# Reordering the start: tile 1's first state in step 1, products within tiles 0 and 1 by even and odd heads, a gate subtraction behind the finishes

## Chip, cores and metric
One core of one Trainium2 chip runs the whole program in one launch. The metric is the device time of a launch in microseconds; lower is better. Engines: TensorE multiplies matrices (PE in profile rows, PEld its weight loads), VectorE (DVE) and ScalarE (ACT) work elementwise, GpSimd (POOL) does elementwise work and masks, SyncE (SP) issues the DMAs.

## The reference
Three layers in a row, all in float32. The first is a gated linear recurrence over 768 positions for 2 batches of 8 heads of width 40:

```
m_new = max(f_t + m, i_t)
C = exp(f_t + m - m_new) * C + exp(i_t - m_new) * v_t k_t^T
n = exp(f_t + m - m_new) * n + exp(i_t - m_new) * k_t
y_t = sigmoid(o_t) * (C q_t) / max(|n . q_t|, 1)
```

The second scales y (1536 tokens of 320 numbers) by its inverse root mean square and a gain, and computes `(silu(x @ w_gate) * (x @ w_val)) @ w_out` with an inner width of 1536. The third is `leaky(x @ w_in) @ w_out` with an inner width of 2048 and a slope of 0.01 for negatives.

## The kernel before
The tokens are cut into 12 tiles of 128, n = 0 to 11, two of them (one for each batch) for each stretch of 128 positions. Tiles 0 and 1 are the first of their batch and have no earlier state. The recurrence is done by chunks. For a tile, the score products `k q^T` of each head (`scores`, L1092) are multiplied by a table of decays (VectorE, L802), and `within` (L1131) multiplies that by the values. Each tile also leaves a state (`update_state`, L1121), which later tiles of its batch use (`from_state`). VectorE divides by the denominator (`denominator`, L841 to L844, and `finish`, L850 and L855), ScalarE squares and normalises (L574, L580, with an inverse root on GpSimd, L456, between them), and TensorE turns the tile (`turn`, L1144 and L1147) into the layout in which the second layer reads it. VectorE and ScalarE split the turned values into a high and a low part (`x_hi`, `x_lo`, `x_odd`; L863 to L888, L589, L596), since products are done in a format of fewer bits.

The second layer is a list of steps (`STEPS`), each a block of 128 of the 1536 inner columns for 2 or 4 tiles. Step s has `gate(s)` and `value(s)`, eight products each of 256 or 512 columns (L1166), then tanh on ScalarE (`first1`, L619), `gated` (L908), `hidden1` (L915), `high1` (L633) and `low1` (L929) on VectorE and ScalarE, and `out1` on TensorE (L1205, L1209) one or two steps later. Steps 0 to 9 are for tiles 0 and 1. The recurrence of tiles 2 to 11 runs beside the steps, at places that the table `BESIDE` gives: tile 2's scores go before gate(2).

The weights come by DMA into a ring of three tiles (`raw`), ScalarE rounds them into the high part (L613, `hi_weights`), and GpSimd subtracts to get the low part (L483, L485, `lo_weights`). gate(s) waits for its low part.

Each engine has one hand-written order, and semaphores join them. In the start, TensorE has: exponents of tiles 0 and 1, scores(0), scores(1), within(0), within(1), two tables of gate sums for the later tiles (`table`, L1056: five transposes each of 16 rows), update_state(0), the last rows of the sums (L1270), turn(0), turn(1), update_state(1), gate(0), value(0), gate(1), value(1). The tables land in PSUM and are taken by `later_tables` on VectorE: L780 copies the sums into `a_tab`, L783 subtracts them and gives `c_tab`, which ScalarE's decays of tile 2 on need (L551). L968 makes the input of the second table; it stands on VectorE between the last score product of tile 1 and the first denominator.

`p_done` counts the score products of VectorE, two for each tile: z = 0 for the even heads, z = 1 for the odd. `dc_done` counts the state updates, `tab_ps` the tables in PSUM, `tab_done` the tables in SBUF, `exp_tab` the exponentials of them, `a_done` the gate sums, `gate_used` the runs of `gated`. The states of tiles 0 and 1 lie in two parts of the PSUM bank `c_ps`; `first_state` copies them to SBUF (L821), and scores(2), which write `c_ps` too, wait for both copies. SyncE loads the q and k of tile n into the place of tile n - 2 and waits for `dc_done` n - 1 before it.

Of the kernel before, what the change touches and what calls it, by code (L numbers as in the profile page):

```python
# [8 lines left out]
ALU = mybir.AluOpType  # L9
# [6 lines left out]
SEQ_TILES = S // P  # L16
# [75 lines left out]
def build(nc, first_gates, gates, qk, tok, w1, w2, consts, scratch, out):  # L92
    ctx = ExitStack()
    with ctx:
# [213 lines left out]
        def width(s):  # L308
            return STEPS[s][1] * P if s < STEPS1 else CHUNK
# [229 lines left out]
        def _(act):  # L539
# [131 lines left out]
            nc.scalar.activation(ea_tab[:, NG:], a_tab[:, NG:], ACT.Exp).then_inc(exp_tab, 1)  # L671
            act.wait_ge(tab_ps, 4)
            for z in range(2):
# [65 lines left out]
        def _(dve):  # L739
# [37 lines left out]

            def later_tables():
                dve.wait_ge(tab_ps, 2)
                nc.vector.tensor_copy(a_tab[:, NG:], later_a_ps).then_inc(tab_done, 1)  # L780
                dve.wait_ge(tab_ps, 3)
                dve.wait_ge(tab_done, 2)
                nc.vector.tensor_tensor(c_tab[:, NG:], later_c_ps, a_tab[:, NG:], ALU.subtract).then_inc(tab_done, 1)  # L783
# [31 lines left out]
            def first_state(n):  # L815


                dve.wait_ge(dc_done, FIRST)
# [146 lines left out]
            for n in range(FIRST):  # L965
                for z in range(2):
                    scores(n, z)
            nc.vector.tensor_tensor(ig[0:NG, rest], ig[0:NG, rest], m, ALU.subtract).then_inc(a_done, 1)  # L968
            for n in range(FIRST):
                denominator(n)  # L970
                finish(n)
            later_tables()
            first_x_high()
# [3 lines left out]
            first_state(0)  # L977
            first_state(1)

# [3 lines left out]
            for s in range(1, STEPS1 + 1):  # L983
# [5 lines left out]
                if s < STEPS1:  # L989
                    gated(s, width(s))  # L990
                if h_first(s):
                    hidden1(s, width(s))
# [58 lines left out]
        def _(pe):  # L1051
# [74 lines left out]
            def within(n):  # L1126
                pe.wait_ge(tok_in[n % 2], 16 * (n // 2 + 1))
                pe.wait_ge(p_done, 2 * n + 2)
                for h in range(H):
# [135 lines left out]
            table(later_a_ps, acum, 1, SEQ_TILES)  # L1265
            pe.wait_ge(a_done, 4)
            table(later_c_ps, ig, 1, SEQ_TILES)
            update_state(0)
            pe.wait_ge(tab_done, 3)
# [3 lines left out]
            update_state(1)  # L1273

            gate(0)
            value(0)
            for s in range(1, STEPS1 + 1):
# [3 lines left out]
                if s < STEPS1:  # L1281
                    gate(s)
                for n in work["R"]:
                    from_state(n)
                    within(n)
                    update_state(n)
# [6 lines left out]
                if s == RING:  # L1293

                    pe.wait_ge(exp_tab, 2)
                for ready in outs(s):
                    out1(ready)
# [71 lines left out]
```

## Time and profile before

| | |
|---|---|
| time, median of 3 runs | 440.34 us (439.75 to 440.49) |
| the profiled execution | 440.19 us, span 438.5 us |
| TensorE busy | 429.8 us, 98% of the span |
| VectorE, ScalarE, GpSimd busy | 226.3, 193.3, 91.0 us |

The span runs from the first to the last recorded work of the profiled execution; the rest of its own time lies around the span. All rows below are of that one execution, and times in them count from the start of the span. A timeline row gives the start, the duration of the merged group, the engine, the line, the operation, what it writes and reads, and, in brackets, how long the engine idled before it and what ended the wait. Ends of TensorE's rows are modelled, and neighbouring products overlap, so spacings are taken from starts.

### The profile page before, as it was taken

To read this page: it belongs to the slowest core of one execution; us is meant where nothing else is said; L and a number is where in the kernel's file an instruction comes from. 1 tells how busy PE (TensorE), PEld (TensorE's weight loads), DVE (VectorE), ACT (ScalarE), POOL (GpSimd) and SP (SyncE) were. 2 spreads that over 40 slices of the span, in tenths; PEclk is the share of its full clock that TensorE was granted. 3 is DMA by queue.
4 is the path that set the end of the run, shared out by engine and by line. 5 is a ranking of instruction groups with operands and counts; after the bars stand their busy time and mean duration, and the time that the engine had idled before them with its cause. 6 is when DMAs were issued, how large, how long until landed. Compare 5 with 4: busy or idle time off the path is not lost.

```text
span 438.5 us, 8229 instructions
## 1 busy us (share of the span) xinstructions
PE 429.8 (98%) x3237; PEld 377.7 (86%) x3237; DVE 226.3 (52%) x439; ACT 193.3 (44%) x428; POOL 91.0 (21%) x97
## 2 busy tenths in 40 slices
PE   7999999999999999999999999999999999999997
PEld 5889999999788888878888888989999999999996
DVE  8856656775466555456433335353333333533534
ACT  4867753665262535235333226553343343333332
POOL 1798852212111111002333004430000000000000
PEclk9999999999999999999999999999999999999999
DMA  7887623431202410001222102300000000100101
GB/s 213 279 294 257 215 86 124 126 121 51 78 27 98 131 47 0 1 1 33 66 67 66 34 1 67 100 0 1 0 1 0 1 1 1 44 17 0 61 0 60
DMA packets 10692, 30.42 MB, mean 69 GB/s; under 512 B 1296, under 2 KB 3264, under 8 KB 10656
## 3 DMA queue, kind: packets, MB, share of 16 engines
q1 hardware_dynamic: 10656, 29.92, 21.4%
q8 instruction: 25, 0.41, 0.4%
q14 instruction: 11, 0.09, 0.1%
HBM read 27.90 MB, written 2.01 MB: 68 GB/s over the span
## 4 chain that ended last, share of the span: by engine, by line
PE 82%; issue 6%; POOL 4%; DMA 4%; DVE 3%; ACT 1%; SPq 0%; POOLq 0%; DVEq 0%
PE gate_ps L1166 22%; PE value_ps L1166 22%; PE out_ps L1243 9%; PE out_ps L1205 9%; PE turn_ps L1243 6%; PE out_ps L1209 3%; PE c_ps L1243 3%; PE turn_ps L1131 3%; POOL w_sb L483 2%; DMA raw<-in_w 2%; PE turn_ps L1092 1%; DMA att_sb<-in_tok 1%; PE turn_ps L1109 1%; PE c_ps L1121 1%; DMA y_acc<-in_first_gates 1%
## 5 line engine op out<-in xcount | busy, mean ns | idle before, releaser
L1166 PE MATMUL value_ps<-x_hi,w_sb 128*128 128x512 f32 (+1 forms) x280 | 68.6, 367 | 0.5 <-DVE h_lo L929 0.5
L1166 PE MATMUL gate_ps<-x_hi,w_sb 128*128 128x512 f32 (+1 forms) x280 | 68.8, 368 | 0.2
L1166 PEld LDWEIGHTS gate_ps<-x_hi,w_sb 128*128 128x128 f32 x280 | 47.4, 191 | 8.2 <-DVE x_odd L895 1.1
L1166 PEld LDWEIGHTS value_ps<-x_hi,w_sb 128*128 128x128 f32 x280 | 47.7, 191 | 7.4 <-DVE h_lo L929 0.7
L908 DVE SCALAR_TENSOR_TENSOR act_buf<-act_buf,gate_ps 128x512 f32<-128x512 f32 (+1 forms) x46 | 26.2, 569 | 48.1 <-ACT act_buf L619 47.9
L934 DVE TENSOR_TENSOR h_lo<-hid,h_hi 128x512 fp32r<-128x512 f32 x48 | 33.2, 692 | 33.7 <-ACT h_hi L638 33.7
L633 ACT ACTIVATE h_hi<-value_ps 128x512 fp32r<-128x512 f32 (+1 forms) x46 | 23.0, 500 | 58.4 <-DVE value_ps L915 58.2
L1205 PE MATMUL out_ps<-h_hi,w_sb 128*128 128x512 f32 (+1 forms) x184 | 48.2, 348 | 0.0
L638 ACT ACTIVATE h_hi<-hid 128x512 fp32r<-128x512 f32 x48 | 30.3, 632 | 37.6 <-DVE hid L922 36.5
L619 ACT ACTIVATE act_buf<-gate_ps 128x512 f32<-128x512 f32 (+1 forms) x46 | 23.1, 501 | 49.3 <-PE gate_ps L1166 49.1
L1243 PE MATMUL out_ps<-w_sb,h_hi 128*128 128x320 f32 x192 | 43.0, 309 | 0.2 <-DVE h_lo L934 0.2
L491 POOL TENSOR_TENSOR w_sb<-raw,w_sb 128x704 fp32r<-128x704 f32 x16 | 27.4, 1716 | 76.0 <-ACT w_sb L613 76.0
L1166 PE MATMUL gate_ps<-x_lo,w_sb 128*128 128x512 f32 (+1 forms) x140 | 39.3, 362 | 0.0
L1166 PE MATMUL value_ps<-x_lo,w_sb 128*128 128x512 f32 (+1 forms) x140 | 39.2, 362 | 0.0
L1166 PE MATMUL gate_ps<-x_odd,w_sb 128*128 128x512 f32 (+1 forms) x140 | 39.1, 361 | 0.0
L1166 PE MATMUL value_ps<-x_odd,w_sb 128*128 128x512 f32 (+1 forms) x140 | 39.0, 360 | 0.0
L915 DVE SCALAR_TENSOR_TENSOR value_ps<-act_buf,value_ps 128x512 f32<-128x512 f32 (+1 forms) x46 | 26.5, 577 | 22.2 <-PE value_ps L1166 22.0
L929 DVE TENSOR_TENSOR h_lo<-value_ps,h_hi 128x512 fp32r<-128x512 f32 (+1 forms) x46 | 26.5, 575 | 19.7 <-ACT h_hi L633 19.5
L1205 PEld LDWEIGHTS out_ps<-h_hi,w_sb 128*128 128x128 f32 x184 | 31.7, 190 | 3.8
L922 DVE SCALAR_TENSOR_TENSOR hid<-gate_ps,act_buf 128x512 f32<-128x512 f32 x24 | 16.6, 691 | 34.7 <-ACT act_buf L626 34.7
L1243 PEld LDWEIGHTS out_ps<-w_sb,h_hi 128*128 128x128 f32 x192 | 32.7, 188 | 1.8 <-DVE h_lo L934 0.6
L922 DVE SCALAR_TENSOR_TENSOR hid<-value_ps,act_buf 128x512 f32<-128x512 f32 x24 | 16.6, 691 | 30.4 <-ACT act_buf L626 30.4
(148 smaller groups left out, 797.5 us busy)
## 6 DMA issues: line engine op xcount, KB each, us to landing
raw<-in_w SPq DMA_DIRECT2D x12, 544.0 KB, 4.6
att_sb<-in_tok SPq DMA_DIRECT2D x12, 484.0 KB, 4.8
raw<-in_w SPq DMA_DIRECT2D x16, 352.0 KB, 3.0
expo<-decay_scratch SPq DMA_DIRECT2D x10, 512.0 KB, 5.3
att_sb<-in_qk SPq DMA_DIRECT2D x24, 160.0 KB
out_y<-y_acc SPq DMA_DIRECT2D x12, 160.0 KB, 1.9
consts_sb<-in_consts SPq DMA_DIRECT2D x1, 129.5 KB, 2.7
y_acc<-in_first_gates SPq DMA_DIRECT2D x1, 112.0 KB, 2.6
```

The lines of the kernel that those rows point to most:

```text
L491: nc.gpsimd.tensor_tensor(w[:, W2RAW:W2], r, w[:, 0:W2RAW].bitcast(F32), ALU.subtract).then_inc(w_lo, 1)
L619: nc.scalar.activation(act_buf[:, s % RING, 0:n], gate_ps[:, 0:n], ACT.Tanh, scale=0.5)\
L633: nc.scalar.activation(h_hi[:, r, cols], value_ps[:, 0:width(s)], ACT.Copy).then_inc(hi_done, 1)
L638: nc.scalar.activation(h_hi[:, r, :], hid[:, r, :], ACT.Copy).then_inc(hi_done, 1)
L908: nc.vector.scalar_tensor_tensor(out=a, in0=a, scalar=1.0, in1=gate_ps[:, 0:n], op0=ALU.add, op1=ALU.mult).then_inc(gate_used, 1)
L915: nc.vector.scalar_tensor_tensor(out=value_ps[:, 0:n], in0=act_buf[:, s % 2, 0:n], scalar=0.5, in1=value_ps[:, 0:n], op0=ALU.mult, op1=ALU ...
L922: nc.vector.scalar_tensor_tensor(out=hid[:, r, :], in0=in_ps[r][:, :], scalar=0.01, in1=act_buf[:, r, :], op0=ALU.mult, op1=ALU.max)\
L929: nc.vector.tensor_tensor(h_lo[:, r, cols], value_ps[:, 0:width(s)], h_hi[:, r, cols].bitcast(F32), ALU.subtract).then_inc(h_done, 1)
L934: nc.vector.tensor_tensor(h_lo[:, r, :], hid[:, r, :], h_hi[:, r, :].bitcast(F32), ALU.subtract).then_inc(h_done, 1)
L1166: last = nc.tensor.matmul(ps[:, 0:n], lhs, rhs, start=(j == 0), stop=(j == len(xs) - 1))
L1205: nc.tensor.matmul(out_ps[k][:, cols], lhs, rhs[:, r, place], start=(f == 0 and t == 0 and j == 0), stop=(f == NF1 - 1 and j == 2))
L1243: ins = nc.tensor.matmul(y_ps(i, k)[:, 0:DM], lhs[:, r, tok], rhs, start=(f == 0 and j == 0), stop=(f == GF - 1 and j == 2))
```

## The change
On TensorE, `within` of tiles 0 and 1 goes through the even heads first and waits only for the first score product of its tile, then through the odd heads behind the second. `update_state(1)` moves from before gate(0) to between gate(1) and value(1). The second table, of `later_c`, moves from behind the first one to between gate(0) and value(0), and waits there for `exp_tab`, since it shares a bank with the last rows. These waited for three tables in SBUF and now wait for two.

On VectorE, L968 moves behind the finishes of both tiles and the copy of `a_tab`. `later_tables` is cut in two: `later_sums` stays, `later_gates` goes behind the copy of tile 0's state. That copy waits for tile 0's update alone, and tile 1's copy moves behind gated(1) in step 1. TensorE's wait for `c_tab` moves to before the first `out1`, which writes into that bank.

```
--- before.py
+++ after.py
@@ -669,7 +669,7 @@
             x_high(1)
             act.wait_ge(tab_done, 2)
             nc.scalar.activation(ea_tab[:, NG:], a_tab[:, NG:], ACT.Exp).then_inc(exp_tab, 1)
-            act.wait_ge(tab_ps, 4)
+            act.wait_ge(tab_ps, 3)
             for z in range(2):
                 rows = slice(z * HP, (z + 1) * HP)
                 logs = later_last_ps[rows, :].rearrange("p (m z) -> p z m", z=2)[:, z, :]
@@ -775,10 +775,12 @@
             nc.vector.tensor_tensor_scan(acum[0:NG, rest], restart[0:NG, rest], f, 0.0, ALU.mult, ALU.add)\
                 .then_inc(a_done, 1)
 
-            def later_tables():
+            def later_sums():
                 dve.wait_ge(tab_ps, 2)
                 nc.vector.tensor_copy(a_tab[:, NG:], later_a_ps).then_inc(tab_done, 1)
-                dve.wait_ge(tab_ps, 3)
+
+            def later_gates():
+                dve.wait_ge(tab_ps, 4)
                 dve.wait_ge(tab_done, 2)
                 nc.vector.tensor_tensor(c_tab[:, NG:], later_c_ps, a_tab[:, NG:], ALU.subtract).then_inc(tab_done, 1)
 
@@ -814,8 +816,7 @@
 
             def first_state(n):
 
-
-                dve.wait_ge(dc_done, FIRST)
+                dve.wait_ge(dc_done, n + 1)
                 for p in range(2):
                     rows = slice(p * HP, p * HP + D)
                     ins = nc.vector.tensor_copy(state[rows, n, :], state_ps(n)[rows, 0:PAIRS * DV])
@@ -965,17 +966,17 @@
             for n in range(FIRST):
                 for z in range(2):
                     scores(n, z)
-            nc.vector.tensor_tensor(ig[0:NG, rest], ig[0:NG, rest], m, ALU.subtract).then_inc(a_done, 1)
             for n in range(FIRST):
                 denominator(n)
                 finish(n)
-            later_tables()
+            later_sums()
+            nc.vector.tensor_tensor(ig[0:NG, rest], ig[0:NG, rest], m, ALU.subtract).then_inc(a_done, 1)
             first_x_high()
             for n in range(FIRST):
                 x_low_main(n)
             first_low_odd()
             first_state(0)
-            first_state(1)
+            later_gates()
 
             gated(0, width(0))
             hidden1(0, width(0))
@@ -988,6 +989,8 @@
                     denominator(n)
                 if s < STEPS1:
                     gated(s, width(s))
+                if s == 1:
+                    first_state(1)
                 if h_first(s):
                     hidden1(s, width(s))
                 for n in work["O"]:
@@ -1125,8 +1128,13 @@
 
             def within(n):
                 pe.wait_ge(tok_in[n % 2], 16 * (n // 2 + 1))
-                pe.wait_ge(p_done, 2 * n + 2)
-                for h in range(H):
+                if n >= FIRST:
+                    pe.wait_ge(p_done, 2 * n + 2)
+
+                heads = [*range(0, H, 2), *range(1, H, 2)] if n < FIRST else range(H)
+                for i, h in enumerate(heads):
+                    if n < FIRST and i % PAIRS == 0:
+                        pe.wait_ge(p_done, 2 * n + i // PAIRS + 1)
                     for t0 in range(0, P, HP):
                         last = nc.tensor.matmul(within_ps(n)[t0:t0 + HP, h * DV:(h + 1) * DV],
                                                 expo[:, n % EXPO, h * P + t0:h * P + t0 + HP],
@@ -1263,16 +1271,17 @@
             within(1)
             pe.wait_ge(a_done, 3)
             table(later_a_ps, acum, 1, SEQ_TILES)
-            pe.wait_ge(a_done, 4)
-            table(later_c_ps, ig, 1, SEQ_TILES)
             update_state(0)
-            pe.wait_ge(tab_done, 3)
+            pe.wait_ge(tab_done, 2)
             nc.tensor.matmul(later_last_ps, last_row_sb, a_tab[:, NG:], start=True, stop=True).then_inc(tab_ps, 1)
             turn(0)
             turn(1)
-            update_state(1)
 
             gate(0)
+            pe.wait_ge(a_done, 4)
+
+            pe.wait_ge(exp_tab, 2)
+            table(later_c_ps, ig, 1, SEQ_TILES)
             value(0)
             for s in range(1, STEPS1 + 1):
                 work = beside(s - 1)
@@ -1280,6 +1289,9 @@
                     scores(n)
                 if s < STEPS1:
                     gate(s)
+                if s == 1:
+
+                    update_state(1)
                 for n in work["R"]:
                     from_state(n)
                     within(n)
@@ -1293,6 +1305,7 @@
                 if s == RING:
 
                     pe.wait_ge(exp_tab, 2)
+                    pe.wait_ge(tab_done, 3)
                 for ready in outs(s):
                     out1(ready)
             for g in range(GROUPS):
```

## Rows read from the trace of the kernel before

**Rows 1.** Busy time by stretch: span, each engine, PEclk, DMA share, GB/s
```profile
20.50:24.00 3.50, 3.50 (x20) 3.46 (x17) 2.84 (x9) 2.81 (x9) 3.50 (x4) 1.00 0.98 314
...
27.00:438.40 411.40, 407.42 (x3022) 358.73 (x3020) 205.77 (x387) 175.50 (x381) 75.32 (x72) 1.00 0.18 57
```

**Rows 2.** Timeline of GpSimd: start us, us, operation, [idle before it]
```profile
16.64 0.54 POOL L456 TENSOR_TENSOR ms<-ms,minus_half 128x1 f32<-128x1 f32 x1
...
20.63 0.33 POOL L485 TENSOR_TENSOR w_sb<-raw,w_sb 128x64 fp32r<-128x64 f32 x1
```

**Rows 3.** Timeline of TensorE, 9 to 34 us
```profile
11.93 3.64 PE L1131 MATMUL turn_ps<-att_sb,expo 128*64 128x41 f32 x64 [0.58 <-DVE expo L802]
15.50 1.24 PE L1056 MATMUL out_ps<-consts_sb,y_acc 16*128 16x16 f32 x10
...
19.48 0.42 PE L1147 MATMUL value_ps<-consts_sb,xn 128*64 128x128 f32 x1
19.84 0.78 PE L1121 MATMUL c_ps<-att_sb,kw 128*40 128x41 f32 x16
20.54 1.23 PE L1166 MATMUL gate_ps<-x_hi,w_sb 128*128 128x256 f32 x4
...
22.42 1.06 PE L1166 MATMUL value_ps<-x_hi,w_sb 128*128 128x256 f32 x4
...
24.02 0.64 PE L1166 MATMUL gate_ps<-x_hi,w_sb 128*128 128x256 f32 x4
...
25.65 0.74 PE L1166 MATMUL value_ps<-x_hi,w_sb 128*128 128x256 f32 x4 [0.52 <-DVE h_lo L929]
...
26.80 0.37 PE L1092 MATMUL turn_ps<-att_sb 40*128 40x128 f32 x1
...
33.48 0.49 PE L1121 MATMUL c_ps<-att_sb,kw 128*40 128x41 f32 x16
```

**Rows 4.** Timeline of ScalarE
```profile
15.63 0.47 ACT L574 ACTIVATE xn<-yt 128x321 f32<-128x321 f32 x1 [0.38 <-DVE yt L855]
...
17.63 0.55 ACT L580 ACTIVATE xn<-yt,ms 128x320 f32<-128x320 f32 x1
...
20.48 0.39 ACT L676 ACTIVATE dec_tab<-out_ps 64x40 f32<-64x40 f32 x2
...
22.94 1.27 ACT L551 ACTIVATE expo<-expo,c_tab 128x128 f32<-128x128 f32 x4
```

**Rows 5.** Timeline of VectorE
```profile
11.09 0.69 DVE L802 TENSOR_TENSOR expo<-expo,gate_ps 128x512 f32<-128x512 f32 x1
...
13.33 0.84 DVE L968 TENSOR_TENSOR y_acc<-y_acc 16x640 f32<-16x640 f32 x1
...
16.63 0.49 DVE L855 TENSOR_TENSOR yt<-turn_ps,den 128x320 f32<-128x320 f32 x1
...
17.38 0.24 DVE L783 TENSOR_TENSOR c_tab<-out_ps,a_tab 128x80 f32<-128x80 f32 x1
19.24 0.61 DVE L863 TENSOR_SCALAR x_hi<-out_ps,consts_sb 128x128 fp32r<-128x128 f32 x2 [1.62 <-PE value_ps L1147]
...
21.17 0.48 DVE L888 SCALAR_TENSOR_TENSOR x_odd<-value_ps,consts_sb,x_odd 64x256 fp32r<-64x256 f32 x1
21.68 1.36 DVE L821 COPY state<-c_ps 40x164 f32<-40x164 f32 x4
...
25.59 0.42 DVE L908 SCALAR_TENSOR_TENSOR act_buf<-act_buf,gate_ps 128x256 f32<-128x256 f32 x1
```

**Rows 6.** DMA issued from 10.4 to 11.2 us: count, size, median us to landing
```profile
raw<-in_w SPq DMA_DIRECT2D x1, 544.0 KB, 4.9
```

**Rows 7.** Timeline of SyncE's DMA issues
```profile
10.61 0.43 SPq L374 DMA_DIRECT2D raw<-in_w  x1
...
25.13 0.68 SPq L352 DMA_DIRECT2D att_sb<-in_qk  x2
...
27.32 4.74 SPq L374 DMA_DIRECT2D raw<-in_w  x2
```

More of the change, by code:

```diff
@@ L671, in _ @@
             nc.scalar.activation(ea_tab[:, NG:], a_tab[:, NG:], ACT.Exp).then_inc(exp_tab, 1)
-            act.wait_ge(tab_ps, 4)
+            act.wait_ge(tab_ps, 3)
             for z in range(2):
@@ L776, in _, with later_sums, later_gates @@
                 .then_inc(a_done, 1)
-            def later_tables():
+            def later_sums():
                 dve.wait_ge(tab_ps, 2)
                 nc.vector.tensor_copy(a_tab[:, NG:], later_a_ps).then_inc(tab_done, 1)
-                dve.wait_ge(tab_ps, 3)
+            def later_gates():
+                dve.wait_ge(tab_ps, 4)
                 dve.wait_ge(tab_done, 2)
@@ L815, in first_state @@
             def first_state(n):
-                dve.wait_ge(dc_done, FIRST)
+                dve.wait_ge(dc_done, n + 1)
                 for p in range(2):
@@ L967, in _ @@
                     scores(n, z)
-            nc.vector.tensor_tensor(ig[0:NG, rest], ig[0:NG, rest], m, ALU.subtract).then_inc(a_done, 1)
             for n in range(FIRST):
@@ L971, in _ @@
                 finish(n)
-            later_tables()
+            later_sums()
+            nc.vector.tensor_tensor(ig[0:NG, rest], ig[0:NG, rest], m, ALU.subtract).then_inc(a_done, 1)
             first_x_high()
@@ L977, in _ @@
             first_state(0)
-            first_state(1)
+            later_gates()
             gated(0, width(0))
@@ L990, in _ @@
                     gated(s, width(s))
+                if s == 1:
+                    first_state(1)
                 if h_first(s):
@@ L1127, in within @@
                 pe.wait_ge(tok_in[n % 2], 16 * (n // 2 + 1))
-                pe.wait_ge(p_done, 2 * n + 2)
-                for h in range(H):
+                if n >= FIRST:
+                    pe.wait_ge(p_done, 2 * n + 2)
+                heads = [*range(0, H, 2), *range(1, H, 2)] if n < FIRST else range(H)
+                for i, h in enumerate(heads):
+                    if n < FIRST and i % PAIRS == 0:
+                        pe.wait_ge(p_done, 2 * n + i // PAIRS + 1)
                     for t0 in range(0, P, HP):
@@ L1265, in _ @@
             table(later_a_ps, acum, 1, SEQ_TILES)
-            pe.wait_ge(a_done, 4)
-            table(later_c_ps, ig, 1, SEQ_TILES)
             update_state(0)
-            pe.wait_ge(tab_done, 3)
+            pe.wait_ge(tab_done, 2)
             nc.tensor.matmul(later_last_ps, last_row_sb, a_tab[:, NG:], start=True, stop=True).then_inc(tab_ps, 1)
@@ L1272, in _ @@
             turn(1)
-            update_state(1)
             gate(0)
+            pe.wait_ge(a_done, 4)
+            pe.wait_ge(exp_tab, 2)
+            table(later_c_ps, ig, 1, SEQ_TILES)
             value(0)
@@ L1282, in _ @@
                     gate(s)
+                if s == 1:
+                    update_state(1)
                 for n in work["R"]:
@@ L1295, in _ @@
                     pe.wait_ge(exp_tab, 2)
+                    pe.wait_ge(tab_done, 3)
                 for ready in outs(s):
```

## Prediction

> **What bounds the kernel now.** I read the table of stretches first. From 27 us to the end TensorE is busy for 407.42 of 411.40 us, so whatever happens at the start moves the end by as much as it moves TensorE's first steps, and by nothing more [rows 1]. Behind 27 us it runs through its steps almost without a stop. The weights are no limit either: the weights of `gate(1)` are split by GpSimd at 20.96 and TensorE asks for them at 24.02, 3 us later [rows 2, 3]. So the question is only when the first `gate`/`value` pair and the chain behind it come.
>
> The timeline of TensorE shows the start as a relay. It stands idle for 0.58 and starts `within` at 11.93, when VectorE has both score products of tile 0, and is done with both tiles at 15.57. After the turns (the last one starts at 19.48) it does `update_state(1)` from 19.84, gate(0) from 20.54, value(0) from 22.42, gate(1) from 24.02, and then stands idle for 0.52 before value(1) at 25.65, waiting for VectorE's low part of step 0 [rows 3]. ScalarE's timeline shows why the turns come when they do: behind `hi_weights(1)` it idles 0.38, to 15.63, for tile 0's y, and from there square, weights, square, normalise, normalise run one behind the other up to the last turn [rows 4].
>
> **The clock.** The column of the granted clock reads 1.00 before 24 us and behind 27 alike [rows 1], but four products of 256 columns take 1.06 in value(0) and 0.64 in gate(1) [rows 3]: 0.42 less over three spacings, so 0.213 against about 0.12 each. The first is 256 columns at the 1.2 GHz level, the second nearly that at 2.4 GHz. The rise comes at about 24.0, after 3.5 us in which TensorE did full 128 by 128 products without a pause; `within`, tables and turns before ran at the lower level.
>
> **The change, part by part.**
>
> 1. `within` by even and odd heads. The 64 records take 3.64 us either way. The even heads need only the first product, which is over before the second begins at 11.09 [rows 5], so TensorE can use the 0.58 that it idled: start at 11.35, done at 14.99. The odd heads need the second product (11.78) and come to their turn at 12.26, a quarter of 3.64 later. Bounds: 0 to 0.84 (11.93 less 11.09); I take 0.58, the idle time of the row.
>
> 2. VectorE subtracts behind the finishes. L968 (13.33 to 14.17) leaves the place between the last product and the denominators, so up to 0.84 of VectorE goes ahead of the finishes; but tile 1's needs `within(1)`, so I take the 0.58 of part 1: its y ends at 16.54 instead of 17.12. L968 now lies between about 16.8 and 17.7, inside the 1.62 that VectorE idled until 19.24 for the turned tile [rows 5]; without that cover it would cost 0.84.
>
> 3. What of it reaches the turns. ScalarE is busy with `hi_weights(1)` until 15.25 (15.63 less 0.38), so tile 0's square gains only that idle 0.38 [rows 4]. Behind it come `hi_weights(2)`, whose raw tile was issued at 10.61 and lands 4.9 later, at 15.5 [rows 6, 7], in time for its turn at 15.7 (15.25 and 0.47 for the square), and then square(1) at about 16.8, for which y is ready at 16.54. GpSimd's inverse root for tile 0 ends at 17.18, being held by its own weights [rows 2]; normalise(0), at 17.63 before [rows 4], wants it at 17.25. So 0.38 of the 0.58 passes, and the last turn starts at 19.10.
>
> 4. `update_state(1)` leaves the place before gate(0): 0.70 of TensorE (19.84 to 20.54). But gate(0) then meets its operands. VectorE's chain of low parts ends with L888 at 21.17 + 0.48 = 21.65 [rows 5], which becomes 21.27; gate(0)'s last two products need it, so they start at 21.33, and with 0.05 for the restart gate(0) has issued all at about 21.8. Of 1.08 (0.38 + 0.70) some 0.6 is left. Bounds: 0.38 (only the shift) to 1.08 (no wait for operands), the row of L888 decides.
>
> 5. `table(later_c)` goes between gate(0) and value(0). Ten transposes of both tables take 1.24 at the low clock [rows 3], so five take 0.62, and I add 0.1 for the two changes of kind. In the old place they were hidden, since TensorE waited for normalise afterwards; here they are in front of value(0). The sum: 21.8 + 0.7 = 22.5, against 22.42. Bounds 0.31 (higher clock) to 0.9. Its own waits, for the subtraction (17.7) and for the last-row exponentials (20.87 before, [rows 4], 20.5 now), are satisfied.
>
> 6. `later_gates` (0.24, [rows 5]) follows tile 0's state copies on VectorE: L821 took 1.36 for both tiles, 0.68 for one, so 21.3 to 22.0, then it waits for the table, 22.6 to 22.85. Queued behind it is gated(0), at about 22.9 instead of 23.04 (21.68 + 1.36); the ScalarE decay of tile 2 that needs the c table started at 22.94 [rows 4] and would start about then. Cost 0; a table 0.3 later would begin to delay gated(0), which gate(1) waits for only at 24.0.
>
> 7. `update_state(1)` goes between gate(1) and value(1), in TensorE's idle 0.52. At the higher clock a state update is 0.49 [rows 3], at the lower 0.78. Cost 0 to 0.3; I take 0, as value(1) waits for VectorE's low part until 25.65 anyway. VectorE copies the state behind gated(1) (25.59 + 0.42 = 26.01), to 26.7, while TensorE is in value(1); scores(2), which need that copy, start at 26.80 [rows 3, 5]. Margin 0.1, cost 0 to 0.1.
>
> 8. SyncE: tile 3's q and k wait for the second state update. They went out at 25.13 [rows 7], now at about 25.8, and the issue after them (27.32, weights) waits for GpSimd and not for them. Cost 0.
>
> The sum at value(0) is +0.1 us, and with nothing later changed also at the end. The profiled execution took 440.19 (span 438.5, 1.7 outside it), 0.15 under the median of 440.34. So 440.3 for the execution, 440.4 for the median.
>
> **A rule weighed against the rows.** The rows show five transposes newly placed in the stretch of full products after which the clock rises [rows 3]. The Trainium skill (TensorE: Matmul & The Clock Gate, Part 4) says that PE transposes do not bring TensorE to its full clock as products do. By it this change thins the very work that releases the clock; by the rows alone the rise stays at 24.0. The result of this rule is the first rival, and no row of this trace can confirm it.
>
> **Rivals.**
>
> *The clock rises later (slower).* Place: gate(0) now has pauses for operands, and 0.7 us of small transposes follow it, where before there were 3.5 us of unbroken full products. For it: the mixed work from 11.9 to 20.5 never raised the clock. Against: TensorE is still hardly idle. Price: gate(1) from 24.1 with eight products at 0.213 (1.7), the state update (0.7) and value(1) (1.7) end at 28.2 instead of 26.8: +1.4, so 441.8; the idle 0.52 before value(1) is counted in it. It decides (over 0.88) from a rise later than about 26.5, when over eight products that nothing hides cost 0.093 more each.
>
> *The clock rises earlier (faster).* `within` now follows the scores without the 0.58 pause, so scores, products and tables make one unbroken run. If this, or the earlier gate(0), brings the higher clock by 21.3, then the two last products take 0.24, the table 0.31 and 0.1, value(0) 0.96: it is issued at 22.95 instead of 24.02, less 1.07: 439.3. Against: 3.6 us of `within` without a pause did not do it before.
>
> *The clock follows gate(0) by the same distance as before.* Gate(0) starts 0.85 earlier (19.7, ScalarE's and VectorE's high parts of tile 1 being the 0.38 earlier), so the rise is at 23.1: of value(0)'s products some six, and not the last one or two, save 0.093 each, 0.5; with +0.1 and the median, 440.0.
>
> *The change doesn't do what it says at the front.* TensorE may not start the even heads early, or ScalarE's weights be late: the 0.38 is lost, the table stays: +0.5, 440.8.
>
> **How the numbers follow.** Within 0.2% is 0.88 us, about what a measurement of this kernel can tell. Forecast 0.36 (439.9 to 440.9 by the bounds of parts 4, 5 and 7), clock follows 0.12, front not gained 0.06: together 0.54 within. Clock later 0.24, slower. Clock earlier, or more of the 1.08 of part 4 passing with it, 0.22, faster. The range 439.1 to 441.8 reaches to both outer cases and leaves out their far tails, some 0.15.
>
> **What the profile after would show.** Right: `within` at 11.3 or before, the last turn near 19.1, gate(0) from about 19.7 with a pause before its low products, the table near 21.9, value(0) at 22.5, value(1) near 25.7, and full products at 0.12 from 24.0. Wrong in part 3: the last turn at 18.8 or 19.4. Wrong in part 5: value(0) at 22.1 or before. The number itself fails above all if the spacing of 0.213 ends somewhere else than at 24.0.

## The result, and the profile after

The changed kernel takes 442.45 us (median of 7 runs, 441.34 to 442.80), the kernel before 440.34 in the same measurement: a ratio of 1.0046, with an interval of 1.0036 to 1.0056. It is 2.1 us slower. The forecast was 440.4, the range ended at 441.8. The profiled execution took 442.8, span 441.1.

The table of stretches of the changed kernel, with the columns of [rows 1]:

```profile
20.50:24.00 3.50, 3.50 (x16) 2.96 (x17) 2.59 (x9) 2.35 (x7) 3.50 (x4) 1.00 0.93 280
24.00:29.00 5.00, 5.00 (x37) 4.69 (x37) 1.85 (x6) 3.15 (x11) 3.45 (x4) 1.00 0.79 288
29.00:441.00 412.00, 407.99 (x3026) 358.98 (x3025) 205.87 (x387) 175.52 (x381) 75.19 (x71) 1.00 0.18 56
```

Behind 29 us TensorE is idle for 4.01 us, as it was for 3.98 behind 27 us before [rows 1]. Nothing was lost or won there: the whole difference lies ahead of scores(2). The timeline of TensorE, with the rows that answer to [rows 3]:

```profile
12.03 3.64 PE L1139 MATMUL turn_ps<-att_sb,expo 128*64 128x41 f32 x64
15.60 0.71 PE L1059 MATMUL out_ps<-consts_sb,y_acc 16*128 16x16 f32 x5
...
19.70 0.42 PE L1155 MATMUL value_ps<-consts_sb,xn 128*64 128x128 f32 x1
20.30 1.19 PE L1174 MATMUL gate_ps<-x_hi,w_sb 128*128 128x256 f32 x4 [0.18 <-ACT x_hi L589]
21.46 0.79 PE L1174 MATMUL gate_ps<-x_lo,w_sb 128*128 128x256 f32 x2
22.05 0.71 PE L1174 MATMUL gate_ps<-x_odd,w_sb 128*128 128x256 f32 x2
22.70 0.71 PE L1059 MATMUL out_ps<-consts_sb,y_acc 16*128 16x16 f32 x5
23.34 1.22 PE L1174 MATMUL value_ps<-x_hi,w_sb 128*128 128x256 f32 x4
...
25.21 1.05 PE L1174 MATMUL gate_ps<-x_hi,w_sb 128*128 128x256 f32 x4
...
27.05 0.78 PE L1124 MATMUL c_ps<-att_sb,kw 128*40 128x41 f32 x16
27.76 1.22 PE L1174 MATMUL value_ps<-x_hi,w_sb 128*128 128x256 f32 x4
28.78 0.44 PE L1174 MATMUL value_ps<-x_lo,w_sb 128*128 128x256 f32 x2
...
29.38 0.37 PE L1095 MATMUL turn_ps<-att_sb 40*128 40x128 f32 x1
```

From start to start, after against [rows 3]: gate(0) begins 0.24 earlier; gate(0) to value(0) takes 3.04 instead of 1.88 (+1.16); value(0) to gate(1) 1.87 instead of 1.60 (+0.27); gate(1) to value(1) 2.55 instead of 1.63 (+0.92); value(1) to scores(2) 1.62 instead of 1.15 (+0.47). The sum is +2.58, and the span grew by 2.6.

Four products of 256 columns take 1.05 to 1.22 everywhere from gate(0) to value(1). Before, gate(1) was the first to take 0.64 [rows 3]. The spacing of 0.213, 256 columns at the 1.2 GHz level, now ends in the low products of value(1), at about 28.9 instead of 24.0. The granted clock column reads 1.00 all the while, as it did before, but the trace holds no record of the clock for that time: its first record, at full, begins at 28.86 here and at 23.88 before. The spacings and the first record put the rise at the same place.

The rows that answer to [rows 5] are those of VectorE:

```profile
17.30 0.85 DVE L973 TENSOR_TENSOR y_acc<-y_acc 16x640 f32<-16x640 f32 x1
...
21.44 0.48 DVE L889 SCALAR_TENSOR_TENSOR x_odd<-value_ps,consts_sb,x_odd 64x256 fp32r<-64x256 f32 x1
21.95 0.67 DVE L822 COPY state<-c_ps 40x164 f32<-40x164 f32 x2
23.45 0.24 DVE L785 TENSOR_TENSOR c_tab<-out_ps,a_tab 128x80 f32<-128x80 f32 x1 [0.83 <-PE out_ps L1059]
```

VectorE works in the order that the prediction said, the subtraction some 0.5 later than it said. But `x_odd` ends at 21.92, later than before (21.65), and not at 21.27. In this execution the start itself was late: ScalarE's first half of `raw` waited 0.84 for its DMA and began at 13.44, and GpSimd's inverse root came at 17.30 instead of 16.64:

```profile
17.30 1.27 POOL L456 TENSOR_TENSOR ms<-ms,minus_half 128x1 f32<-128x1 f32 x2
```

That is why I ran the same kernel twice more (below).

### The profile page after: what moved, and what is told of

Its sections match the earlier page's. It is cut to its first block, busy times and chain, and to the rows that moved or that the text cites. A ratio compares the mean times of both kernels' runs of the same rounds, so it can differ in the third digit from the quotient of the medians.

```text
span 441.1 us, 8230 instructions
## 1 busy us (share of the span) xinstructions
PE 432.2 (98%) x3237; PEld 379.0 (86%) x3237; DVE 226.5 (51%) x439; ACT 193.4 (44%) x428; POOL 91.2 (21%) x97
## 4 chain that ended last, share of the span: by engine, by line
PE 82%; issue 6%; POOL 5%; DMA 2%; ACT 2%; DVE 2%; SPq 1%; POOLq 0%; DVEq 0%; ACTq 0%
PE gate_ps L1174 23%; PE value_ps L1174 23%; PE out_ps L1251 9%; PE out_ps L1213 9%; PE turn_ps L1251 6%; PE out_ps L1217 3%; POOL w_sb L483 3%; PE c_ps L1251 3%; DMA raw<-in_w 2%; PE turn_ps L1139 2%; PE turn_ps L1095 1%; PE turn_ps L1112 1%; PE c_ps L1124 1%; POOL w_sb L485 1%; ACT w_sb L613 1%
## 5 line engine op out<-in xcount | busy, mean ns | idle before, releaser
L916 DVE SCALAR_TENSOR_TENSOR value_ps<-act_buf,value_ps 128x512 f32<-128x512 f32 (+1 forms) x46 | 26.6, 577 | 22.9 <-PE value_ps L1174 22.7
L930 DVE TENSOR_TENSOR h_lo<-value_ps,h_hi 128x512 fp32r<-128x512 f32 (+1 forms) x46 | 26.5, 575 | 19.2 <-ACT h_hi L633 18.9
```

Of the source, the lines that this page charges most:

```text
L916: nc.vector.scalar_tensor_tensor(out=value_ps[:, 0:n], in0=act_buf[:, s % 2, 0:n], scalar=0.5, in1=value_ps[:, 0:n], op0=ALU.mult, op1=ALU ...
L930: nc.vector.tensor_tensor(h_lo[:, r, cols], value_ps[:, 0:width(s)], h_hi[:, r, cols].bitcast(F32), ALU.subtract).then_inc(h_done, 1)
```

## The experiments

Three theories: the clock rises later because the small table products stand between gate(0) and value(0) (A in the expectations); or it is the work itself, table, restarts, late operands and state update, at any clock; or the subtraction moved on VectorE disturbs someone else (C in the expectations). The time of the kernel before beside each run was measured together with it. Execution times of one kernel mostly spread by 1 to 3 us, so ratios with their intervals decide, and rows of one execution show only what was possible in it.

**1. The same products, two kinds.** Into the kernel before, between gate(0) and value(0), five unneeded transposes (a repeat of the second table), or three unneeded full products of about the same length. The outputs don't change.

```
             gate(0)
+            pe.wait_ge(exp_tab, 2)
+            table(later_c_ps, ig, 1, SEQ_TILES)
             value(0)
```

> The kernel before, with five more transposes of the second table between gate(0) and value(0) (a second copy of work already done). Theory A, the clock: small transposes break the stretch of full products, the spacing of 0.213 us lasts beyond 24.9 us, and the time grows by 1.3 to 2.5 us. Theory B, only work: the 0.65 us of transposes are added in front of value(0) and nothing else, so +0.6 to +0.8 us, with the spacing of 0.12 from about 24 us.

Measured: 441.22 beside 440.19, ratio 1.0023 (1.0009 to 1.0037), runs from 439.67 to 442.36. That lies between what the two theories expected, and the interval doesn't tell them apart.

```
             gate(0)
+            for _ in range(3):
+                nc.tensor.matmul(out_ps[0][:, 0:FIRST * P], w1_sb[:, 0, 0:P], x_hi[:, 0, FIRST_TOK],
+                                 start=True, stop=True)
             value(0)
```

> The kernel before, with three full products of 256 columns, not used by anything, in the place where e1 has its transposes: about the same 0.64 us of TensorE. Theory A: the stretch of full products is unbroken, the clock rises at about 24 us, and the time grows by 0.4 to 0.7 us (the last products of value(0) are then at the higher clock). Theory B: the same as the transposes, within 0.2 us of e1.

Measured: 440.48, ratio 1.0005 (0.9994 to 1.0016). The medians lean the way of the clock theory (+1.0 against +0.3, the second a little less than either theory expected), but the intervals overlap. The profiled execution of the first is one of its quicker ones (440.35), and there the clock had risen before the transposes began:

```profile
20.77 1.17 PE L1166 MATMUL gate_ps<-x_hi,w_sb 128*128 128x256 f32 x4
21.78 0.40 PE L1166 MATMUL gate_ps<-x_lo,w_sb 128*128 128x256 f32 x2
...
22.41 0.48 PE L1056 MATMUL out_ps<-consts_sb,y_acc 16*128 16x16 f32 x5
22.81 0.74 PE L1166 MATMUL value_ps<-x_hi,w_sb 128*128 128x256 f32 x4
```

The rise is in gate(0), at about 21.8, and the transposes start at 22.41, so in this execution they can't have put it off; its slower executions have no profile. The pair agrees in direction with the rule of the Trainium skill that the prediction weighed (TensorE: Matmul & The Clock Gate, Part 4), but doesn't prove it. It also changes two things at once: the transposes are of 16 columns and the products of 256, and no run here tells whether it matters that they are transposes or that they are small.

**2. The parts one by one.** The state update of tile 1 alone (both engines' parts of it, into the kernel before), `within` by even and odd heads alone, the moves of the table and the subtraction alone; then the change without the moves of table and subtraction, and the change with the state update put back. The edits are the matching lines of the diff, done or undone. Their core on TensorE (an excerpt, with remarks added):

```
# update alone / within alone / gates alone, into the kernel before
-            update_state(1)          # before gate(0)
+                if s == 1:
+                    update_state(1)  # behind gate(1)
...
+                heads = [*range(0, H, 2), *range(1, H, 2)] if n < FIRST else range(H)
...
             gate(0)
+            pe.wait_ge(a_done, 4)
+            pe.wait_ge(exp_tab, 2)
+            table(later_c_ps, ig, 1, SEQ_TILES)
             value(0)
```

> The kernel before, with only update_state(1) and first_state(1) moved to step 1. Theory A: gate(0) has pauses for its operands, from 21.4 us on the full products are unbroken as far as value(1)'s state update; the rise may slip by some us, which makes it +0.5 to +1.5 us; if it does not slip, value(0) comes 0.3 earlier and the time falls by 0.2 to 0.5. Theory B: -0.2 to -0.5 us, since value(0) starts at about 22.1 in place of 22.42.

> The kernel before, with only the even and odd heads of within(0) and within(1). Both theories: within(0) starts up to 0.58 us earlier, but the finish of tile 0 waits for VectorE's subtraction (ends 14.17), so nothing passes on: 0 within 0.2 us. The clock rises at about 24 us unless the unbroken run at 8 to 16 us brings it up earlier; then -1 us.

> Only the move of the gate sums: VectorE subtracts behind the finishes, the table goes between gate(0) and value(0), both states stay before gate(0). Theory A, the clock: as e1 (a table in the stretch of full products), so +0.7 to +1.5 us, with single times spread over 2 us or more. Theory B, work in front of value(0): the 0.65 us of the table less what the earlier finishes give (0.4), so +0.2 to +0.3 us.

> The change without the move of the gate sums: even and odd heads, and update_state(1) with its copy in step 1. Theory A: the stretch from gate(0) to the end of gate(1) is unbroken but for short pauses, so the clock mostly rises by 25 us: 0 to +0.5 us, as e3. Theory B: the same as e3 within 0.2, since the split of the heads is covered by VectorE's subtraction.

> The change with update_state(1) and both state copies back before gate(0). Theory A in its strong form (the table before value(0) and the state update after gate(1) leave only value(0) and gate(1) unbroken, too short a stretch): without the second break the clock rises in more of the executions, so +0.7 to +1.5 us in place of the +2.0 of the whole change. Theory B: the part of the 2.0 us that update_state(1) makes is 0.1 to 0.3 us, so still +1.7 us or more.

| kernel | median us | before | ratio (interval) |
|---|---|---|---|
| state update alone | 440.50 | 440.19 | 1.0008 (0.9996 to 1.0020) |
| within alone | 439.93 | 440.19 | 1.0000 (0.9990 to 1.0011) |
| gates alone | 441.78 | 440.20 | 1.0033 (1.0020 to 1.0047) |
| change without the gates | 440.65 | 440.20 | 1.0012 (1.0003 to 1.0021) |
| change with the update back | 441.81 | 440.20 | 1.0042 (1.0025 to 1.0058) |

The moves around the table cost 1.6 alone, more than either theory expected; within the change they are the difference between 440.65 and 442.45. Every kernel that has them is slower by 0.3 to 0.5%, those without them by about 0.1% at most. The state update alone did not bring the 0.2 to 0.5 less that the work theory expected. The kernel with the update back (1.0042) is not to be told from the changed one (1.0046), so the second break, by the state update, is not shown to cost anything in time. The timeline of TensorE with the gates alone:

```profile
22.29 0.71 PE L1058 MATMUL out_ps<-consts_sb,y_acc 16*128 16x16 f32 x5
22.93 1.22 PE L1168 MATMUL value_ps<-x_hi,w_sb 128*128 128x256 f32 x4
...
24.80 1.05 PE L1168 MATMUL gate_ps<-x_hi,w_sb 128*128 128x256 f32 x4
...
26.48 0.74 PE L1168 MATMUL value_ps<-x_hi,w_sb 128*128 128x256 f32 x4
```

The low clock lasts until about 26.3 here, through gate(1). A late rise is not all that these kernels lose by. The profiled execution with the update back (441.09) has the table between the blocks too, yet its clock rose at 22.34, in gate(0) and ahead of the table; it was late already, with the first turn at 18.96 instead of 18.23 and gate(0) at 21.14 instead of 20.54 (experiment 5 shows what held the turns). And the change without the gates has its rise at 25.28, 1.4 later than before, with no table between. `within` alone starts at 11.19 instead of 11.93, and its first turn only 0.11 earlier (18.12): tile 0's y still waits for the subtraction that stands ahead of the denominators.

**3. The clock taken out of it.** Sixteen unneeded products of 512 columns (bf16) ahead of gate(0), in the kernel before and in the changed one, so that both do gate(0) and all behind it at the upper level. The outputs don't change.

```
+            for _ in range(16):
+                nc.tensor.matmul(gate_ps[:, :].rearrange("p (q t) -> p q t", q=PAIRS), unit[:, :],
+                                 unseen[:, :].unsqueeze(1).broadcast_to([P, PAIRS, P]), start=True, stop=True)
             gate(0)
```

> The kernel before, with 16 full products of 512 columns, not used by anything, ahead of gate(0): 6.8 us at the lower level, so that the clock has risen when gate(0) begins. By all theories the time grows by the fill less what gate(0) and value(0) gain at the higher level (1.5 us): +3 to +5.5 us. It is the ruler for the run beside it, in its rows from gate(0) to the scores of tile 2 above all.

> The changed kernel with the same fill ahead of gate(0). Theory A, the clock: what made the change slow was the lower level lasting longer; with the clock up in both kernels this one is at most 0.5 us slower than the filled kernel before, and from gate(0) to the scores of tile 2 the rows differ by the table, 0.3 to 0.4 us, alone. Theory B, work and waits: still 1.5 to 2 us slower than the filled kernel before.

Measured: 442.72 (ratio to before 1.0064, 1.0051 to 1.0077) and 443.70 (1.0083, 1.0070 to 1.0096), beside 439.79. The timelines of TensorE, first before with the fill, then after with it:

```profile
20.51 3.85 PE L1276 MATMUL gate_ps<-unseen,unit 128*128 128x512 bf16 x16
24.01 0.82 PE L1166 MATMUL gate_ps<-x_hi,w_sb 128*128 128x256 f32 x4
...
25.15 0.64 PE L1166 MATMUL value_ps<-x_hi,w_sb 128*128 128x256 f32 x4
...
28.88 0.37 PE L1092 MATMUL turn_ps<-att_sb 40*128 40x128 f32 x1
```

```profile
18.69 5.30 PE L1281 MATMUL gate_ps<-unseen,unit 128*128 128x512 bf16 x16
23.64 0.83 PE L1174 MATMUL gate_ps<-x_hi,w_sb 128*128 128x256 f32 x4
...
24.88 0.48 PE L1059 MATMUL out_ps<-consts_sb,y_acc 16*128 16x16 f32 x5
25.29 0.74 PE L1174 MATMUL value_ps<-x_hi,w_sb 128*128 128x256 f32 x4
...
29.13 0.37 PE L1095 MATMUL turn_ps<-att_sb 40*128 40x128 f32 x1
```

From gate(0) to scores(2) the two take 4.87 and 5.49: the change costs 0.62 there at the upper level, 0.51 of it for the table and its restarts (1.65 less 1.14 to value(0)), 0.11 for all from there to scores(2), the moved state update among it. That is the share of the work itself. In the unfilled pair the same stretch is 6.26 and 9.08, 2.82 more; 2.2 of it goes with the lower clock and with late operands. The stretch from value(0) on separates these two, since there the changed kernel waits for no operand: it takes 1.66 more in the unfilled pair (6.04 against 4.38) and 0.11 more in the filled pair (3.84 against 3.73). So about 1.5 us goes with the clock alone.

But the expectation for the times failed: the medians of the filled kernels still differ by 0.98, not by half a microsecond. The profiles don't show why. In the changed kernel the fill took longer (4.95 to gate(0) against 3.50), most of it at the lower level: the granted clock is 0.50 from 18.96 to 22.38. But it also began 1.82 earlier, and these two executions took the same time (442.64 and 442.69); the slower ones of the changed kernel, up to 444.42, have no profile.

**4. The subtraction back, and the table before gate(0).** From the changed kernel: L973 back in its old place; or the table ahead of gate(0) and `hi_weights(2)` behind both normalises.

```
+            nc.vector.tensor_tensor(ig[0:NG, rest], ig[0:NG, rest], m, ALU.subtract).then_inc(a_done, 1)
             for n in range(FIRST):
...
             later_sums()
-            nc.vector.tensor_tensor(ig[0:NG, rest], ig[0:NG, rest], m, ALU.subtract).then_inc(a_done, 1)
```

> The changed kernel with only VectorE's subtraction back in front of the first denominators. Theory C, a collision: behind the finishes the subtraction runs beside GpSimd's low weights and inverse roots, where a GpSimd row of 0.32 us was seen to take 0.91; then this kernel is 0.2 to 0.6 us faster than the changed one (441.9 to 442.2). Theories A and B: the finishes come later by up to 0.7 us and ScalarE takes that up, so the same as the changed kernel within 0.2 us (442.3 to 442.6).

Measured: 442.44, ratio 1.0050 (1.0037 to 1.0063): the same time as the changed kernel. The gain of 0.2 to 0.6 that theory C expected did not come.

```
-            hi_weights(2)            # ScalarE, between the squares
...
+            hi_weights(2)            # behind normalise(1)
...
+            pe.wait_ge(a_done, 4)
+            table(later_c_ps, ig, 1, SEQ_TILES)
             gate(0)
```

> The changed kernel with the table moved from behind gate(0) to in front of it, where TensorE waits for operands, and the third tile's high weights behind both normalises on ScalarE. Theory A: gate(0), value(0) and gate(1) are one stretch of full products again and value(0) starts at 21.8 to 22.2: 439.4 to 440.3 us, at or below the kernel before. Theory B: the table is out of the path between gate(0) and value(0), 0.7 us less than the changed kernel: 441.5 to 441.9.

Measured: 440.46 beside 439.79, ratio 1.0016 (1.0006 to 1.0025). Most of the loss is gone, more than the work theory expected (441.5 to 441.9). Which of the two edits did it was open, so the table was moved alone. In both runs the waits that its shared bank asks for move with it: ScalarE's last rows wait for the table too, and `later_gates` waits for them.

> The changed kernel with nothing but the table moved from behind gate(0) to in front of it (with the waits that sharing its bank asks for). TensorE waits there for tile 1's high parts anyway, so gate(0) comes 0.3 later and value(0) 0.4 to 0.6 earlier. Theory A, the clock: gate(0), value(0) and gate(1) are one stretch, so 1.2 to 1.8 us less than the changed kernel: 440.2 to 441.0, near the run without the gate move (440.65). Theory B, work: only the 0.4 to 0.6 us: 441.8 to 442.1.

Measured: 440.90 beside 440.38, ratio 1.0003 (0.9984 to 1.0022). One move of five small products takes back the loss: its interval lies wholly below the changed kernel's. The clock theory had expected 440.2 to 441.0, the work theory 441.8 to 442.1, which its interval excludes (0.9984 to 1.0022 is 439.7 to 441.3). The timeline of TensorE:

```profile
20.25 0.71 PE L1060 MATMUL out_ps<-consts_sb,y_acc 16*128 16x16 f32 x5
20.89 1.22 PE L1175 MATMUL gate_ps<-x_hi,w_sb 128*128 128x256 f32 x4
...
22.85 1.05 PE L1175 MATMUL value_ps<-x_hi,w_sb 128*128 128x256 f32 x4
...
26.67 0.74 PE L1175 MATMUL value_ps<-x_hi,w_sb 128*128 128x256 f32 x4
...
27.86 0.34 PE L1096 MATMUL turn_ps<-att_sb 40*128 40x128 f32 x1
```

Here gate(0) starts 0.59 later than in the changed kernel, and value(0) 0.49 earlier, for gate(0) meets its operands ready and nothing stands behind it. The spacing of 0.213 ends at about 26, in gate(1): 2.4 to 3.7 earlier than in the changed kernel, but still 2 later than in the kernel before. Last, with this kernel as the base, the subtraction put back as well:

> The run with only the table moved, and besides VectorE's subtraction back in front of the first denominators. Theory C, the collision with GpSimd's inverse roots and low weights on its way to the turns: the turns come 0.3 to 0.6 earlier and the time is 0.3 to 0.6 less than with the subtraction behind the finishes, beside the same runs of the kernel before. Rival: the finishes then come later by up to 0.7 and take the gain back, no difference within 0.2.

Measured: 440.69 beside 440.20, ratio 1.0008 (0.9999 to 1.0017). As in the first pair, putting it back changes nothing that can be measured; the intervals would hide up to half a microsecond.

**5. The changed kernel twice more**, for the spread of the rise and to see whom the subtraction meets.

> The changed kernel once more, for the time at which the spacing of 0.213 us ends in one more execution. Theory A: between 25.5 and 29 us, and the execution's time goes with it: late rise, long time. Theory B: no relation, and value(1) is late by the same 2 us whenever the clock rises.

> The same kernel as the run before it, for another execution. Theory A: a rise between 25.5 and 29 us, and a time that goes with it. Theory B: no relation between the two.

Measured: 443.26 and 442.68. From value(0) to scores(2) they take 6.34 and 5.76, the first one 6.04, before 4.38; the spacing changes at about 29.6 and 28.4. The late rise was no accident of one execution. The times go with it, as the clock theory expected: with the rise at 28.3, 28.4, 28.9 and 29.6 the executions took 442.44 (the one with the subtraction back), 442.68, 442.80 and 443.26. GpSimd and VectorE in the first of the two repeats, then in the second:

```profile
14.23 2.36 POOL L483 TENSOR_TENSOR w_sb<-raw,w_sb 128x1024 fp32r<-128x1024 f32 x1 [0.78 <-ACT w_sb L613]
16.55 0.92 POOL L485 TENSOR_TENSOR w_sb<-raw,w_sb 128x64 fp32r<-128x64 f32 x1
17.43 1.07 POOL L456 TENSOR_TENSOR ms<-ms,minus_half 128x1 f32<-128x1 f32 x2
```

```profile
16.48 0.80 DVE L973 TENSOR_TENSOR y_acc<-y_acc 16x640 f32<-16x640 f32 x1
```

```profile
16.58 0.31 POOL L485 TENSOR_TENSOR w_sb<-raw,w_sb 128x64 fp32r<-128x64 f32 x1
16.85 1.69 POOL L456 TENSOR_TENSOR ms<-ms,minus_half 128x1 f32<-128x1 f32 x2
```

```profile
16.80 0.80 DVE L973 TENSOR_TENSOR y_acc<-y_acc 16x640 f32<-16x640 f32 x1
```

GpSimd's last 64 columns of the low weights take 0.92 instead of 0.33 [rows 2] in the one, its two inverse roots 1.69 instead of 1.07 in the other; whichever starts just after L973 is 0.6 longer. In the first execution the first inverse root began together with L973 (both at 17.30) and took its usual 0.55; only the second was longer, 0.66. TensorE waits for normalise in both repeats; the rows of the first:

```profile
16.62 0.71 PE L1276 MATMUL out_ps<-a_tab,consts_sb 128*128 128x80 f32 x2 [0.42 <-DVE a_tab L780]
18.63 0.69 PE L1152 MATMUL out_ps<-consts_sb,xn 128*128 128x128 f32 x2 [1.29 <-ACT xn L580]
```

**6. A version that beats the kernel before?** The kernel before with seven unneeded products of 512 columns on ones at the very start; the same with three small ones around the turns (`keep_busy`: 256 columns, two behind `update_state(0)`, one between the turns); and that with the even and odd heads. The outputs don't change.

```
+            pe.wait_ge(ones_set, 1)
+            warm_up(5)
             unseen_tokens()
+            warm_up(2)
...
             update_state(0)
+            keep_busy(2)
...
             turn(0)
+            keep_busy(1)
             turn(1)
```

> The kernel before, with seven more full products of 512 columns on a tile of ones, not used by anything, five before and two behind the products of the unseen tokens, in time in which TensorE waits for the gates. Theory A: the clock is up from about 5 us, the scores and within go faster, and if it stays up through the turns, gate(0) and value(0) save up to 1.5 us: 438.7 to 439.7; if it falls again before gate(0) by the thin work of 16 to 20 us, no change within 0.5. Theory B: no change, or +0.2 us if the products run past 5.1 us.

> The kernel before with the products on ones at the start, as in the warm run, and three more of 256 columns in TensorE's short waits before and between the turns. Theory A: the clock stays up more often through the turns, 439.0 to 439.8; where it does not, the three products delay the turns by up to 0.4. Theory B: +0.2 to +0.4 us.

> The warm and busy run with the even and odd heads of the change besides. The heads alone made no difference, so the same as the warm and busy run: 0.2 to 0.8 us below the kernel before by theory A (the clock up in more of the executions), no difference by theory B.

Measured: 439.75 beside 440.20, ratio 0.9995 (0.9984 to 1.0006); 439.89 beside 440.38, 0.9980 (0.9961 to 1.0000); 440.41 beside 440.20, 1.0009 (0.9998 to 1.0020). The hint of the second did not hold in the third, so no version here is shown to be faster than before. The timeline of TensorE in the second shows why an earlier clock pays so little:

```profile
22.14 0.64 PE L1169 MATMUL value_ps<-x_hi,w_sb 128*128 128x256 f32 x4
...
23.73 0.71 PE L1169 MATMUL gate_ps<-x_hi,w_sb 128*128 128x256 f32 x4 [0.49 <-DVE act_buf L911]
```

value(0) runs at the upper level, and gate(1) then waits 0.49 for VectorE's gated(0), which needs ScalarE's activation of gate(0) first. Even so scores(2) start at 26.13, 0.67 earlier than before, and the span is 438.7, not shorter. The gain is lost at 37.03, where TensorE waits for a low part of VectorE, behind ScalarE, which had waited for weights from the DMA:

```profile
35.13 1.11 ACT L616 ACTIVATE w_sb<-raw 128x1088 fp32r<-128x1088 f32 x1 [2.79 <-DMA raw<-in_w]
37.03 0.74 PE L1169 MATMUL value_ps<-x_hi,w_sb 128*128 128x256 f32 x4 [0.68 <-DVE h_lo L932]
```

In the kernel before, that product starts at 36.87 and its low part ends at 36.59, so an earlier start has only 0.28 to give there.

## Why the prediction was wrong

The step that failed is the sum: "+0.1 us, and with nothing later changed also at the end". Its first half was mis-sized: value(0) started 0.92 later than before (1.05 and 1.10 in the repeats), made of -0.24 for gate(0)'s start, +0.52 for the operands that gate(0) waited for and the restarts, and +0.64 for the table. Its second half left the rise at 24.0 while the work ahead of the rise changed: from value(0) to scores(2) the changed kernel took 1.66 more (1.96 and 1.38).

What came was the first rival, "the clock rises later", to which I gave 0.24; it named the table between gate(0) and value(0) as the place and its condition (a rise later than 26.5) was met (28.4 to 29.6). Its price of 1.4 was for the way from gate(1) to scores(2), 4.1 instead of 2.7, and it was right: 4.17 instead of 2.78. Its total still fell short (441.8 against 442.45), since it stood on the +0.1 at value(0).

That the table's position decides is shown by moving it alone (442.45 to 440.90). That the clock is how it costs time rests on the spacings in every profile, on the filled pair (0.11 left of 1.66 behind value(0)) and on the four executions whose times go with their rises. Why the clock rose later isn't shown as well: with the table ahead of gate(0) it still rose later than in the kernel before (25.5 to 26.0), without any table between it rose at 25.3 once, and with the table between it rose at 21.8 and 22.3 in two kernels that kept `update_state(1)` ahead of gate(0) (in a third at 26.3). How much the transposes, the pauses in gate(0) and the moved state update each do to the rise stays open.

- **Part 1** (0.58 at `within`): `within` began at 11.21 and 11.53 in the two repeats, 0.7 and 0.4 earlier, so the term was right; in the first execution scores(1) waited 0.52 for the DMA of its q and k and `within` began at 12.03.
- **Part 2** (the subtraction costs nothing inside VectorE's 1.62 of idle): the cover was there and the term still wrong in the rows. The work beside it on GpSimd, which holds tile 0's normalise, became 0.6 longer in the two repeats and in the change with the update back (L485 0.91). In time nothing is measured: with it back, 442.44 for 442.45 and 440.69 for 440.90. That what it gives to the finishes and what it takes from GpSimd are of one size isn't shown.
- **Part 3** (0.38 reaches the turns, the last at 19.10): failed. It came at 19.70 to 19.79. I had GpSimd's inverse root end at 17.18 with 0.07 to spare and didn't ask what could lengthen it; in the repeats it begins at 17.43 and 16.85, and normalise at 18.01 and 18.06 instead of 17.63 [rows 4]. In the first execution it was the late weights that held it.
- **Part 4** (gate(0) has issued all at 21.8): mis-sized. The place before gate(0) was won, it starts at 20.30 to 20.40 instead of 20.54, but its low products wait for operands that end at 21.92 to 22.10 and not at 21.27; it has issued all at 22.5 to 22.7. Of the 0.70 taken out nothing is left.
- **Part 5** (the table 0.7): right, 0.64 from its start to value(0)'s. value(0) came at 23.34 to 23.52 for part 4's reason, not at 22.5.
- **Part 6** (`later_gates` 0): right. gated(0) started at 23.61, 0.7 later than forecast, and gate(1) did not wait for it.
- **Part 7** (the state update in an idle gap, 0): taken at 0, it came to 0.2, inside its bounds. At the low clock it fills 0.71 where 0.52 were idle, and the gap is gone: value(1) waits for nobody now. Alone, in the kernel before, the move measured 1.0008 (0.9996 to 1.0020), not to be told from nothing.
- **Part 8** (SyncE 0): right. Tile 3's q and k went out at 27.87 and TensorE's idle time behind 29 us is unchanged.

The rival "the change doesn't do what it says at the front" (0.06) came true in its effect as well, on top of the first: the 0.38 was lost, in the repeats by GpSimd and not by the causes that the rival names. I had priced the cases one at a time, each 0.4 to 1.4, and made the range from single ones; two of them together end outside it, at 442.2.

One premise has a limit that this result didn't touch: that a move at the start moves the end by as much. In 15 of the 20 profiled executions the way from scores(2) to the end of the span is 411.6 to 411.7. With the early clock of experiment 6, in its second kernel, it was 412.6, so the rival "the clock rises earlier" would hardly have given its whole 1.07.

## What to carry to other kernels

In a start where the clock is still low, price a move by what it does to the run of full products around it, not by its own length: in this kernel five transposes of 0.6 us cost some 1.5 us between the first two blocks of products and nothing that could be measured ahead of them. Filling a hole on one engine is free only if nobody on another engine is held by what runs beside it: look at the chain that ends last in that stretch, here GpSimd's. And where two bad cases can hold at once, the range must hold their sum.

## What the runs showed of the hardware

- A GpSimd operation that starts while VectorE's subtraction of two SBUF operands (16x640, 0.80) runs becomes longer: 128x64 from 0.33 to 0.92, the inverse root of 128x1 from 0.54 to 1.17 (the first of the two that take 1.69 together). It ends a fixed time behind the subtraction, as if it had waited for it: the 128x64 at 17.47 for 17.28, 0.19 behind it; the inverse root at 18.02 for 17.60 in the second repeat and at 18.57 for 18.15 in the first execution, 0.42 behind it both times. The one that began together with it took its usual 0.55. With the subtraction in its old place both inverse roots take 0.55. The Trainium skill (GPSIMD Engine Reference, Specifications) says that GpSimd's SBUF interfaces are shared with VectorE, with contention for VectorE instructions in a 2-port mode or with two SBUF inputs. These rows agree with it, as far as contention goes; no run here changed the operands to test it.
- The clock can go up and fall again within the start. The stretches of the kernel before with the warm start, the granted clock third from the end:

```profile
12.00:16.00 4.00, 4.00 (x67) 3.81 (x67) 3.81 (x11) 2.71 (x4) 2.16 (x2) 0.50 0.67 264
16.00:20.00 4.00, 2.94 (x42) 2.18 (x43) 2.53 (x11) 3.30 (x9) 3.68 (x5) 0.93 0.74 278
20.00:24.00 4.00, 4.00 (x35) 3.92 (x30) 3.41 (x12) 3.41 (x11) 4.00 (x4) 0.61 0.95 291
```

It is up in the stretch of `update_state(0)` and the turns, where TensorE is busy for only 2.94 of 4.00, and down again when gate(0) starts, although TensorE is busy throughout from there. Warming the engine early bought nothing measurable.
- The moment of the rise wanders between executions of one kernel: 28.4 to 29.6 in three of the changed one, and the times of one kernel (the one with the transposes added) spread by 2.7 us (439.67 to 442.36).
